# Two chained MLPs after a causal convolution: every TensorE product of the double slots split into two halves of 64 array rows

## The reference, cut to what matters

```python
def reference(x, weight, moe_w_in, moe_w_out, moe2_w_in, moe2_w_out):
    # x: (2, 4096, 192) f32; weight: (8 heads, 7 taps)
    w = softmax(weight, axis=-1)                       # per head, 7 taps
    x_pad = concat([zeros(B, 6, D), x], axis=1)
    x = sum_k w[head, k] * x_pad[:, s + k, head]       # causal convolution, 24 features a head
    x = x.reshape(8192, 192)
    h = x @ moe_w_in                                   # 192 -> 2048
    g = where(h >= 1, h, where(h <= -1, 0, (h + 1) ** 2 / 4))
    y = g @ moe_w_out                                  # 2048 -> 192
    h = y @ moe2_w_in                                  # 192 -> 2048
    g = h * sigmoid(1.702 * h)
    return g @ moe2_w_out                              # 2048 -> 192
```

## Time and profile before

| what | us |
|---|---|
| median of three runs | 1244.41 (1242.61 to 1244.42) |
| the profiled execution | 1242.95 |
| its span in the profile | 1241.0 |
| PE busy | 1216.0 (98%) |
| PEld busy | 1025.4 (83%) |
| DVE busy | 872.7 (70%) |
| ACT busy | 766.4 (62%) |
| POOL busy | 470.1 (38%) |

### The profile page before, as it was taken

How to read it: one execution, slowest core, us unless ns; L and a number is a source line. 1 busy time by engine, 2 the same in 40 slices (tenths; PEclk the granted TensorE clock), 3 DMA queues, 4 the chain that set the end, 5 groups by cost and what they waited for, 6 DMA issues and landing times.

```text
span 1241.0 us, 17811 instructions
## 1 busy us (share of the span) xinstructions
PE 1216.0 (98%) x5928; PEld 1025.4 (83%) x5928; DVE 872.7 (70%) x1221; ACT 766.4 (62%) x1577; POOL 470.1 (38%) x422
## 2 busy tenths in 40 slices
PE   7998999999999999999999999999999999999998
PEld 3777778888888888888888888888888888888887
DVE  6975868677686867768687786867768677665632
ACT  4866675666657566575656757566575656754454
POOL 5858919063270814509063260804408062000000
PEclk8998999999999999999999999999999999999999
DMA  6221010000000000000000000000000000000000
GB/s 170 73 66 58 1 45 4 29 13 32 13 32 0 13 32 13 32 13 12 20 13 32 13 32 0 13 32 13 32 13 25 7 13 2 13 1 1 13 14 13
DMA packets 10655, 29.78 MB, mean 24 GB/s; under 512 B 1028, under 2 KB 5378, under 8 KB 10624
## 3 DMA queue, kind: packets, MB, share of 16 engines
q1 hardware_dynamic: 10624, 29.38, 7.4%
HBM read 23.09 MB, written 6.29 MB: 24 GB/s over the span
## 4 chain that ended last, share of the span: by engine, by line
PE 88%; POOL 7%; ACT 2%; DVE 1%; DMA 1%; issue 1%; SPq 0%; POOLq 0%; ACTq 0%; DVEq 0%
PE acc L597 15%; PE h L502 9%; PE h L504 9%; PE h L503 9%; PE h L505 9%; PE h L506 9%; PE acc L598 7%; PE acc L572 4%; PE acc L577 4%; PE acc L571 4%; PE acc L578 4%; PE acc L575 4%; POOL x_conv L417 3%; POOL prod L410 3%; DMA x_in<-in_x 1%
## 5 line engine op out<-in xcount | busy, mean ns | idle before, releaser
L664 ACT ACTIVATE clip<-clip,half 128x512 f32<-128x512 f32 x256 | 185.4, 724 | 396.3 <-DVE clip L835 396.0
L597 PE MATMUL acc<-w_down,g_hi 128*128 128x384 f32 x1024 | 306.5, 354 | 0.9 <-DVE g_lo L856 0.9
L856 DVE TENSOR_TENSOR g_lo<-gate,g_hi 128x512 fp32r<-128x512 f32 x256 | 207.2, 809 | 87.3 <-ACT gate L680 85.8
L598 PE MATMUL acc<-w_down,g_lo 128*128 128x192 f32 x1024 | 256.6, 251 | 0.0
L844 DVE TENSOR_TENSOR gate<-h,clip 128x512 f32<-128x512 f32 x232 | 160.4, 691 | 136.0 <-ACT clip L664 127.5
L835 DVE TENSOR_SCALAR clip<-h 128x512 f32<-128x512 f32 x244 | 167.5, 687 | 109.7 <-PE h L506 108.4
L410 POOL TENSOR_TENSOR x_conv<-x_in,tap_w 128x384 f32<-128x384 f32 (+2 forms) x30 | 26.1, 890 | 522.9 <-ACT raw L720 519.9
L850 DVE TENSOR_TENSOR g_lo<-gate,g_hi 128x512 fp32r<-128x512 f32 x232 | 217.3, 936 | 4.7 <-ACT g_hi L670 3.6
L417 POOL TENSOR_TENSOR x_conv<-x_conv,prod 128x384 f32<-128x384 f32 (+2 forms) x180 | 206.4, 1166 | 1.6
L410 POOL TENSOR_TENSOR prod<-x_in,tap_w 128x384 f32<-128x384 f32 (+2 forms) x180 | 203.9, 1155 | 8.2 <-DMA x_in<-in_x 3.5
L597 PEld LDWEIGHTS acc<-w_down,g_hi 128*128 128x128 f32 x1024 | 192.3, 188 | 14.3 <-issue 1.6
(11 more groups left out here) (164 smaller groups left out, 2031.6 us busy)
## 6 DMA issues: line engine op xcount, KB each, us to landing
x_in<-in_x SPq DMA_DIRECT2D x14, 960.0 KB, 4.7
out_y<-y_out_a SPq DMA_DIRECT2D x8, 384.0 KB, 2.3
out_y<-y_out_b SPq DMA_DIRECT2D x7, 384.0 KB, 2.4
raw<-in_moe_w_out SPq DMA_DIRECT2D x6, 384.0 KB, 3.4
raw<-in_moe_w_in SPq DMA_DIRECT2D x4, 512.0 KB, 7.4
raw<-in_moe_w_in SPq DMA_DIRECT2D x8, 256.0 KB, 7.1
x_in<-in_x SPq DMA_DIRECT2D x1, 768.0 KB, 4.3
x_in<-in_x SPq DMA_DIRECT2D x2, 283.5 KB
```

What stands on the lines that cost most here:

```text
L597: nc.tensor.matmul(acc2[j][:, 0:2 * D], hi[:, tok], w[:, 0:2 * D], start=first, stop=False)
L598: ins = nc.tensor.matmul(acc2[j][:, D:2 * D], lo[:, tok], w[:, 0:D], start=False, stop=last)
L664: nc.scalar.activation(c, c, ACT.Square, bias=half[:, :], scale=0.5).then_inc(square_ready, 1)
L856: nc.vector.tensor_tensor(g2_lo[k][:, :], gate2[:, :], g2_hi[k][:, :].bitcast(FP32), ALU.subtract).then_inc(g2_lo_ready, 1)
```

## The change

In the double slots no matmul uses all 128 rows of the array. Every product is cut along its contraction into the lower 64 rows (partitions 0 to 63, `LOWER`) and the upper 64 (`UPPER`), and matmuls on the lower rows stand in turn with matmuls on the upper rows, one from each MLP, in different PSUM banks. In the built program these matmuls have a tile of 64 rows by 128 columns at row 0 or row 64.

- **Up.** An up step is now nine half matmuls for each MLP: three main terms on each half, and for rest hi·hi, hi·lo, lo·hi, without lo·lo. They lie in two slots: `begin_up` (four pairs, at the end of the ups of slot n) and `end_up` (five pairs, at the start of slot n+1), since MLP 1 begins on the lower rows and ends on the upper, and MLP 2 the other way round.
- **Down.** `down_both` holds 34 half matmuls: ten of 512 columns (MLP 1) and 24 of 192 (MLP 2). The matmul of 384 columns is now two of 192 onto the same 192 columns of PSUM, so hi and lo are summed there, and two slabs share a bank. Four banks become two (`ACC2_BANKS`), the two others go to h (`h[0]` to `h[3]`, two for each MLP), and `take_out` is two copies of 384 columns on ScalarE and nothing on VectorE.
- **Order and waits.** Downs lag by two (`LAG`) in place of one. TensorE now waits for its own halves (`h1_half`, `h2_half`, `main_half`, `rest_half`, `acc2_half`) before the other rows of the array write the same bank. The alone slots at the end are one more, with `down2` in three matmuls a slab there too. ScalarE puts the first gate of MLP 2 ahead of the square; VectorE takes over the finished tile of MLP 1 before the clip of the slot's step.

```diff
-        h = [ctx.enter_context(nc.psum_tensor(f"h{k}", [P, 512], FP32)) for k in range(2)]
+        h = [ctx.enter_context(nc.psum_tensor(f"h{k}", [P, 512], FP32)) for k in range(4)]
-        acc2 = [ctx.enter_context(nc.psum_tensor(f"acc2_{k}", [P, 512], FP32)) for k in range(4)]
+        acc2 = [ctx.enter_context(nc.psum_tensor(f"acc2_{k}", [P, 512], FP32)) for k in range(2)]
...
+            def begin_up(one, two):
...
+                if isinstance(one.n, int) and one.n < BEHIND + 2:
+                    pe.wait_ge(g1_lo_ready, one.n - SOLO_BANKS + 1)
+                else:
+                    pe.wait_ge(gate1_ready, one.n - 1)
+                nc.tensor.matmul(bank_1, in_hi[0][LOWER, cols1], x_hi[LOWER, :], start=True, stop=False)
...
+                    pe.wait_ge(gate2_ready, two.n - 1)
+                nc.tensor.matmul(bank_2, in_hi[1][UPPER, cols2], y_hi[UPPER, :], start=True, stop=False)
+                nc.tensor.matmul(bank_1, in_hi[0][LOWER, cols1], x_lo[LOWER, :], start=False, stop=False)
+                nc.tensor.matmul(bank_2, in_hi[1][UPPER, cols2], y_lo[UPPER, :], start=False, stop=False)
...
+            def end_up(one, two):
...
+                pe.wait_ge(h1_half, one.n - (BEHIND - 1))
+                nc.tensor.matmul(bank_1, in_hi[0][UPPER, cols1], x_hi[UPPER, :], start=False, stop=False)
+                pe.wait_ge(h2_half, two.n + 1)
+                nc.tensor.matmul(bank_2, in_hi[1][LOWER, cols2], y_hi[LOWER, :], start=False, stop=False)
...
+            def down_both(one, two):
...
+                def slab(j, rows, start, stop):
+                    tok = slice(j * P, (j + 1) * P)
+                    k, at = j // SLABS_PER_BANK, j % SLABS_PER_BANK
+                    dst = acc2[k][:, at * D:(at + 1) * D]
+                    nc.tensor.matmul(dst, hi2[rows, tok], w2[rows, 0:D], start=start and at == 0, stop=False)
+                    nc.tensor.matmul(dst, hi2[rows, tok], w2[rows, D:2 * D], start=False, stop=False)
+                    return nc.tensor.matmul(dst, lo2[rows, tok], w2[rows, 0:D], start=False,
+                                            stop=stop and at == SLABS_PER_BANK - 1)
...
+                nc.tensor.matmul(main[:, :], w_main[LOWER, :], hi1[LOWER, :], start=first1, stop=False)
...
+                slab(0, UPPER, first2, False)
+                nc.tensor.matmul(main[:, :], w_lo[LOWER, :], hi1[LOWER, :], start=False, stop=False)
+                slab(1, UPPER, first2, False).then_inc(acc2_half[0], 1)
...
+                nc.tensor.matmul(rest[:, :], w_rest[LOWER, :], hi1[LOWER, :], start=first1, stop=False)
+                slab(2, UPPER, first2, False)
+                pe.wait_ge(g1_lo_ready, one.n + 1)
+                nc.tensor.matmul(main[:, :], w_main[LOWER, :], lo1[LOWER, :], start=False, stop=False).then_inc(main_half, 1)
+                slab(3, UPPER, first2, False).then_inc(acc2_half[1], 1)
+                nc.tensor.matmul(rest[:, :], w_rest[LOWER, :], lo1[LOWER, :], start=False, stop=False).then_inc(rest_half, 1)
+
+                pe.wait_ge(main_half, one.n - (BEHIND - 1))
+                nc.tensor.matmul(main[:, :], w_main[UPPER, :], hi1[UPPER, :], start=False, stop=False)
+                pe.wait_ge(acc2_half[0], two.n + 1)
+                slab(0, LOWER, False, last2)
...
             def slot(tile, side, s):
...
+                if n is None or n > BEHIND:
+                    end_up(back(tile, side, s, 1), back(tile, side, s, BEHIND + 1))
+                begin_up(back(tile, side, s, 0), back(tile, side, s, BEHIND))
+                if n is None or n >= BEHIND + LAG:
+                    down_both(back(tile, side, s, LAG), back(tile, side, s, BEHIND + LAG))
...
-            def take_out(tile, side):
-                for j in range(SLABS_PER_TILE):
-                    dve.wait_ge(out_copied, tile * SLABS_PER_TILE + (j + 1))
-                    y = y_out[side][:, j, :]
-                    nc.vector.tensor_tensor(y, acc2[j][:, D:2 * D], y, ALU.add).then_inc(out_summed, 1)
```

More of the change, by code:

```diff
@@ L135, in conv_mlp_mlp @@
         h2_ready = sem("h2_ready")
+        h1_half = sem("h1_half")
+        h2_half = sem("h2_half")
+        main_half = sem("main_half")
+        rest_half = sem("rest_half")
+        acc2_half = [sem(f"acc2_half{k}") for k in range(2)]
         g2_hi_ready = sem("g2_hi_ready")
@@ L594, in down2 @@
                     tok = slice(j * P, (j + 1) * P)
[L595 to L600, removed]
+                    k, at = j // SLABS_PER_BANK, j % SLABS_PER_BANK
+                    if at == 0 and first and (not isinstance(step.n, int) or step.tile > 0):
+                        pe.wait_ge(out_copied, step.tile * ACC2_BANKS - (ACC2_BANKS - 1 - k))
+                    dst = acc2[k][:, at * D:(at + 1) * D]
+                    nc.tensor.matmul(dst, hi[:, tok], w[:, 0:D], start=first and at == 0, stop=False)
+                    nc.tensor.matmul(dst, hi[:, tok], w[:, D:2 * D], start=False, stop=False)
+                    ins = nc.tensor.matmul(dst, lo[:, tok], w[:, 0:D], start=False,
+                                           stop=last and at == SLABS_PER_BANK - 1)
+                    if final and at == SLABS_PER_BANK - 1:
+                        ins.then_inc(bank_done, 1)
                 if not final:
@@ L612, in transpose_x, with solo_slot @@
                 ins.then_inc(xT_ready, 1)
-            def slot(tile, side, s):
-                one = back(tile, side, s, 0)
-                two = back(tile, side, s, BEHIND)
[L617 to L630, removed]
+            def solo_slot(tile, side, s):
+                one = back(tile, side, s, 0)
+                if one.n <= AHEAD_FROM:
+                    up1(one)
+                if AHEAD_FROM <= one.n < BEHIND - 1:
+                    up1(back(tile, side, s, -1))
+                if one.n == FIRST_PREP_STEP:
+                    transpose_x(1, acc2)
+                if one.n >= SOLO_LAG:
+                    down1(back(tile, side, s, SOLO_LAG))
+                if one.n == BEHIND - 1:
+                    down1(back(tile, side, s, 1))
+                    down1(one)
@@ L631, in slot, with tail_slot @@
+            def tail_slot(tile, side, s):
+                n = tile * F_TILES + s
+                two = back(tile, side, s, BEHIND)
+                if n == ALL_STEPS:
+                    end_up(back(tile, side, s, 1), back(tile, side, s, BEHIND + 1))
+                    down_both(back(tile, side, s, LAG), back(tile, side, s, BEHIND + LAG))
                 if two is not None:
                     up2(two)
-                if isinstance(tile, int) and tile * F_TILES + s == BEHIND:
-                    for by in range(SOLO_LAG, 1, -1):
-                        down1(back(tile, side, s, by))
@@ L636, in slot @@
[L636 to L642, removed]
+                if n == ALL_STEPS + 1:
+                    down1(back(tile, side, s, LAG))
+                if n > ALL_STEPS:
+                    down2(back(tile, side, s, BEHIND + LAG))
@@ L764, in slot @@
                 two = back(tile, side, s, BEHIND)
+                if two is not None:
+                    gated2(two, 0)
                 if one is not None:
@@ L861, in take_y @@
                 main, rest_acc = acc1
-                upper = slice(DR, P)
+                lower = slice(0, DR)
                 if part == 0:
@@ L918, in slot @@
                     residue1(before1)
+                if takes_y(tile) and not solo and s == 1:
+                    take_y(tile - 1, 1 - side, 0)
+                    take_y(tile - 1, 1 - side, 1)
                 if one is not None:
```

176 lines of the change are left out of this document (119 added, 57 removed).

## The result

| | before | after |
|---|---|---|
| median, us | 1243.51 (1242.09 to 1244.42, 4 runs) | 1263.97 (1262.58 to 1265.9, 4 runs) |
| ratio to before | | 1.0167, 95% interval 1.0148 to 1.0186 |
| profiled execution, us | 1242.95 | 1264.65 |
| its span, us | 1241.0 | 1262.8 |
| double slot, us | 4.64 | 4.71 |

A forecast was written before the change was run, and what follows sets the result against it. TensorE's own issue was taken as the bound. Ups -54, downs +125, ends +4, -1.5 and +1.5 made +75 us on 1242.95: 1318 us, its own range 1295 to 1350, full range with rivals 1205 to 1515.

The forecast's parts named there:

- the rival's 1229: Rival of looser loads or order, 26% together; with a half running ahead of the other and loads at 0.108, 1229 us.
- The bound: Double slots: a slot costs what TensorE needs to issue its own work, 4.64 us before and 4.94 us forecast after.
- Side by side: Two 512-column matmuls on separate row halves take 0.233 us for both, not 0.466 one after the other.
- a load for each half: Weight loads of one row half run beside those of the other, each taking 0.108 us.
- One port: Rival: loads of both halves queue for one port at 0.108 us, `down_both` takes 3.67 us; 1509 us, chance 15%.
- no concurrency: Rival: matmuls on the two halves don't run side by side, 9.1 us a slot, about 2280 us; chance 4%.
- Ups: Up steps: nine pairs, 2.10 us, replace ten matmuls, 2.33 us; gain 0.23 in each of 232 slots, -54 us.
- The price of the 192: Downs of the second MLP: each 192-column matmul costs its weight load, 0.108 us, rather than its columns' 0.0875.
- the order: Each matmul starts behind the one before it in the program, across halves too, so the fifth 512 waits until 1.19 us.
- idle ends: `down_both`: 0.38 us a slot where one array half has nothing to do, within the downs' loss of 0.54, +125 us.
- `main_half`: TensorE's wait at L661 in `down_both`: over at 1.40 us, just inside 1.42, so no cost; 0.06 if loads are quick.
- Ends: Slots outside the double slots: +4 us for second-MLP slots alone, -1.5 at the last down, +1.5 at the 24th slot.

The follow-up runs named there:

- E5: E1 with the dropped lo by lo term of the rest features back as a fifth pair in `begin_up`: 1290.22 us, 1.0381 of the kernel before.
- E3: Kernel before the change, each 384-column matmul of the second MLP's down split into two of 192 on all 128 rows: 1287.82 us, 1.0358 of before.
- E1: The change with the first MLP's third product on main put ahead of the two on rest, in both halves of `down_both`: 1239.74 us, 0.9973 of before.
- E2: The change with all five 512-column matmuls ahead of all twelve of 192 in each half of the downs: 1432.17 us, 1.1517 of before.
- E7: E1 with the downs in coarser turns, two of 512, six of 192, two, six, one: 1241.58 us, 0.9987 of before.
- E8: E1 with the last tile's second-MLP downs in the form before the change, 384 and 192 columns on 128 rows, four banks: 1235.69 us, 0.9946 of before.

## Why the prediction was wrong, point by point

- **The direction** was right by luck. With the order put right and nothing else, the sum falls below the kernel before (the rival's 1229); what made the change slower is a wait of TensorE on itself that I had priced at nothing.
- **The bound.** Right: TensorE's own work, before and after. DVE and ACT stay covered, and no gate leads PE's waits.
- **Side by side, and a load for each half.** Right. Pairs of 512 in 0.233, loads of both halves at the same 704.20. One port (15%) and no concurrency (4%) were out at once.
- **Ups.** Right: -54 us; E5 gives 50.5 for the term dropped.
- **The price of the 192.** Right in kind: it costs its load. 0.108 was a gap between a load and one that had waited for a matmul; loads in a row are 0.111 apart (E3). Twelve times 0.003 is 0.04 us a slot, 8 us too little.
- **The step that failed** is the order: "in the rows each matmul starts behind the one before it in the program, and I keep that across the halves", and so "The fifth matmul of 512 stands behind it in the program, so it can't start before 1.19". It starts at 703.98, 0.93 behind L637, when its own half is free, with two of 192 ahead of it in the program not started. The 0.38 us a slot that I charged for idle ends, 88 us of the +125 for the downs, is not there: without the wait E1 measures 4.600 for the slot, where one half's own matmuls add up to 4.59. All rows before were of one full width, where order and a free array can't be told apart; they could not carry this. The Trainium skill, TensorE: Matmul & The Clock Gate, Part 3: Packing small matmuls — row/col tiling, states the order that I kept. The timeline after shows it broken between the halves (702.91 and 703.00 ahead of 703.05), and the measurement decides. The limit that does exist, three matmuls (E2, E7), costs the turns of the change nothing.
- **`main_half`.** I had it at no cost, "just inside 1.42", because my wrong order had made the turn late. Without it the halves are due 1.16 and 1.18 behind L637 (704.21 and 704.23), but the wait ends at 1.15 and has a load of 0.111 behind it: 0.08 to 0.10 by the timeline, 0.107 a slot and 25 us by E1. In the rival with looser order I had left the wait out; that rival's 1229 plus these 25 and the 8 of the loads is 1262, and 1264 was measured.
- **The sum as it was.** Slot: -0.233 for the dropped term, +0.166 for twelve loads at 0.108 in place of 1.13, +0.036 for 0.111, +0.107 for the wait is +0.076, measured +0.065. The difference is in the slot before, which I summed to 4.63 and which measures 4.642.
- **Ends.** I had +4; measured 6 to 7, of which E8 took 2.3 back by its trace.
- **The range** of 1205 to 1515 held 1264; the forecast's own, 1295 to 1350, did not.

## What to carry to other kernels

Here two halves of the array of 64 rows behaved like two queues: add up one half's own matmuls, each at the longer of its columns (0.233 us for 512, so 0.455 ns each) and its load (0.111 us). Let the program alternate between the halves: a load passed three matmuls that had not started and never four, and turns of one and three or of two and six lost next to nothing by that (E1, E7). Cutting a product in two along its rows saves nothing by itself, it only lets a half-filled product cost half (E5). A matmul narrower than its load, by these two prices some 240 columns (an estimate), costs the load all the same. When one half hands a bank to the other, count 0.45 us from the start of the last matmul on it and put other work between, since the waiting instruction holds up both halves.

## What the runs showed of the hardware that was not expected

- Matmuls of different row halves start out of the program's order: L625 and L626 at 702.91 and 703.00, L637, which stands ahead of both, at 703.05. In E2 the first load of 192 passed three matmuls of 512 that had not started; in E7 one was held for 0.05 us until no more than three were left.
- The load of 64 rows by 128 columns occupies its way into the array for 0.111 us, as that of 128 rows by 128 columns does (E3), and two such loads on different halves start at the same time.
- A matmul's record can open before its load is through: L625 is recorded from 704.21, its load from 704.20, and the next matmul on that half starts only 0.19 later.
